# A fused attention, Fourier, MLP and gated-convolution kernel: the MLP and the value layer on three token blocks of 512 in place of four of 384

## The chip, the cores and the metric

The kernel runs on one core of one Trainium2 chip. The metric is the device time of one execution in microseconds; lower is better.

## The reference, cut to what matters

```python
# 1. causal linear attention with decay, B=2, H=8, S=768, head size 64, chunked
x = attention(q, k, v, lam)                    # (2, 768, 512)
# 2. Fourier mixing, layer norm, MLP
u = x + real(fft(fft(x, axis=1), axis=2))
mu = u.mean(-1); var = ((u - mu) ** 2).mean(-1)
un = (u - mu) / sqrt(var + 1e-6)
y = u + maximum(un @ w_ch1, 0) @ w_ch2         # w_ch1 512x2048, w_ch2 2048x512
# 3. gated convolution
gate = sigmoid(sum(conv_w[k] * shifted(y, k) for k in range(5)))
out = (gate * (y @ w_val)) @ w_out             # (2, 768, 512)
```

There are 2 x 768 = 1536 tokens and 512 features, everything in float32.

## The kernel before, in words

Features lie on the partitions (R = 4 groups of 128) and tokens along the free axis. Every product from the MLP on is made of three matmuls in a reduced form of float32: each operand is split into a high part and a low part (what the high part leaves over), and high x high, high x low and low x high add up in PSUM. ScalarE makes the high parts (a cast), GpSimd the low parts of the weights (`tensor_tensor` subtract), VectorE most of the other low parts.

The work on TensorE falls into stages, in the order in which the program lists them; each engine has its own instruction list and they meet at semaphores.

- Attention of 12 chunks of 128 tokens (6 per batch), with the Fourier transform of batch 0 in between (`hid_transform`, `seq_pair`, `radix4`, `add_pair`).
- `mean(0)`, then `centre` (VectorE subtracts the mean), `cen_hi` (ScalarE) and `cen_lo` (half on VectorE, half on GpSimd) make the MLP's input for batch 0, `cen_h` and `cen_l`.
- The MLP. The 2048 hidden features are worked off in NG = 8 weight groups of 256. A step m is one weight group on one block of TB = 384 tokens (half a batch): `mlp_hidden` has 24 matmuls into PSUM banks 0 and 1, `mlp_out` 24 matmuls into banks 4 to 7, one bank for each R. There are 32 steps, batch 0 first. The two halves of a batch take turns so that a weight group serves two steps; TensorE issues `mlp_hidden` of step m+1 before `mlp_out` of step m. ScalarE applies the Relu (L770) and VectorE makes the low part of the hidden features (L1049) from the same bank. Since the half changes every second step, banks 4 to 7 are emptied every second step: VectorE adds them onto `xT` in SBUF (`add_mlp`, L1064 and L1066).
- Normalization is moved behind the MLP: `finish_mlp` multiplies the sum by 1/std (`rstd`, L337) and adds `u` (L341). `rstd` comes from `squares`, `square_sum`, `variance`, `inverse_roots` and `newton`, spread over the steps, as is the Fourier transform of batch 1 (`hid_transform` 10 and 11, `seq_pair`, `add_pair`, `mean(1)`).
- `value` (48 matmuls for each block of 384 tokens, banks 0 to 3), `gated` (VectorE multiplies by the gate), and `project`, whose moving operand is 512 columns of `w_out` and whose stationary one is 128 tokens.

A weight group is 1 MB in two transfers of 512 KB into `raw_a` or `raw_b`, is split by ScalarE (L735) and GpSimd (L1242) into `w1h`, `w1l`, `w2h`, `w2l` (two buffers, `_a` and `_b`), and is loaded again for batch 1: 16 loads in all. SyncE issues every transfer of the weights and waits for the splits that free the buffer. The batch-1 buffers and `raw_b` overlap the attention's buffers and are free only after the last chunk.

Of the kernel before, what the change touches and what calls it, by code (L numbers as in the profile page):

```python
# [8 lines left out]
F32 = mybir.dt.float32  # L9
# [4 lines left out]
P = 128  # L14
# [3 lines left out]


Step = namedtuple("Step", "m g slot tb rnd first last new fresh")  # L20
# [36 lines left out]
def program(nc, qkv, lam, w_mlp, w_val, conv_w, w_out, seq_tab, hid_tab, out):  # L57
# [13 lines left out]
    TB = S // 2  # L71
    NB = B * 2
    STEPS = 2 * NG
    M = B * STEPS
# [4 lines left out]
    assert (P, Dh, NC, R, K) == (128, 64, 6, 4, 5)  # L79

    with ExitStack() as ctx:
# [28 lines left out]
        cen_h0 = sb("cen_h0", [P, R, S], F32R)  # L110
        cen_l0 = sb("cen_l0", [P, R, S], F32R)
# [14 lines left out]
        with ExitStack() as second:  # L126
# [6 lines left out]
            cen_h1 = sb_in(second, "cen_h1", [P, R, S], F32R)  # L133
        sb("region1_rest", [P, 6 * 2048 + R * PAD])
# [22 lines left out]
        with ExitStack() as second_l:  # L157
            cen_l1 = sb_in(second_l, "cen_l1", [P, R, S], F32R)
# [8 lines left out]
        cen_h, cen_l = [cen_h0, cen_h1], [cen_l0, cen_l1]  # L167
# [18 lines left out]
        s_raw = [sem(f"s_raw{i}") for i in range(2)]  # L186
        s_wh, s_wl = sem("s_wh"), sem("s_wl")
        s_h, s_hh, s_hl, s_ch, s_add, s_scl, s_y = (
            sem(n) for n in ("s_h", "s_hh", "s_hl", "s_ch", "s_add", "s_scl", "s_y"))
# [4 lines left out]

        HID_AT = {0: (10,), 1: (11,)}
        RADIX_AT = {0: (11,)}
# [56 lines left out]
        def group_splits(s):  # L255
            r_ = raw[s]
            half = R * FG
            return [(r_[:, 0:half].rearrange("p (r f) -> p r f", r=R), w1h[s][:, :, :], w1l[s][:, :, :]),
                    (r_[:, half:2 * half].rearrange("p (j r c) -> p j r c", j=2, r=R), w2h[s][:, :, :, :],
                     w2l[s][:, :, :, :])]  # L260

        def value_splits():
            return [(raw[0][:, kk * D:(kk + 1) * D].rearrange("p (r c) -> p r c", r=R), wvh[:, kk], wvl[:, kk])
                    for kk in range(R)]
# [5 lines left out]


        def out_pieces(o):
            if o < NB * 3 - 1:
# [3 lines left out]
        def out_splits():  # L277
            return [(raw[1][:, kk * D:(kk + 1) * D], wo_part(kk, 0), wo_part(kk, 1)) for kk in range(R)]

        GS = len(group_splits(0))  # L280
        GROUPS = B * NG
        AFTER_G = GS * GROUPS
        AFTER_V = AFTER_G + R
        AFTER_O = AFTER_V + R
# [9 lines left out]
        ROUNDS = steps[-1].rnd + 1  # L294
        added_at = {st.tb: st.rnd + 1 for st in steps}
        done_at = {st.tb: st.m + 1 for st in steps}

        def each_step(run):
            for st in steps:
                run(st, steps[st.m + 1] if st.m + 1 < M else None)  # L300

        def tok_half(t, b, hf):
            return t[b][:, :, hf * TB:(hf + 1) * TB]

        def gated_parts(tb):
            if tb == 0:
                return [t[:, :, :, :].rearrange("p a j n -> p (a j) n") for t in (hh, hl)]
            b, hf = divmod(tb - 1, 2)
            return [tok_half(t, b, hf) for t in (cen_h, cen_l)]
# [16 lines left out]

        def finish_mlp(tb, api, eng):

            tt = api.tensor_tensor
            b, hf = divmod(tb, 2)  # L330
            acc, y = tok_half(acc_of, b, hf), tok_half(u, b, hf)
# [1021 lines left out]
```

## Time and profile before

| | |
|---|---|
| median of 3 runs | 432.52 us (432.51 to 433.49) |
| the profiled execution | 432.88 us |
| its span, first to last instruction | 431.1 us |
| TensorE / VectorE / ScalarE / GpSimd busy | 99% / 59% / 37% / 33% |
| MLP steps, first to last matmul | 76.4 to 361.1 us |
| value and projection | 361.1 to 428.5 us |

The busy share of TensorE counts overlapping matmuls, each of which is shown for longer than the distance to the next, so the table tells that it is never idle for long and not how fast it is fed. The distance between the starts of two matmuls is what adds up to the time.

### The profile page before, as it was taken

The numbers are of one execution on the slowest core, as the hardware profiler recorded it, in microseconds if no ns is written. First come the engines' busy times: TensorE is split into PE (matmuls) and PEld (weight loads), VectorE is DVE, ScalarE is ACT, GpSimd is POOL, SyncE is SP. The second block draws the span as 40 slices with busy tenths as digits, with TensorE's granted clock in tenths as the row PEclk, the third lists the DMA queues.
The fourth block names the chain that finished last, engine by engine and source line by source line (L and its number), as shares of the span: only waits on it lengthen the run. The fifth ranks groups of instructions, "written<-read, shape, count | busy, mean of one in ns | idle before, by whom it ended". The sixth has DMA issues, their size and how long they took to land.

```text
span 431.1 us, 7174 instructions
## 1 busy us (share of the span) xinstructions
PE 426.3 (99%) x2914; PEld 409.1 (95%) x2914; DVE 253.1 (59%) x438; ACT 157.5 (37%) x312; POOL 143.6 (33%) x101
## 2 busy tenths in 40 slices
PE   8999999999999999999999999999999999999997
PEld 7888888999999999999999999999999999989986
DVE  5658999682359535435334239937556559899120
ACT  2355843742222411124333163542342261715222
POOL 2553321585332225224664522342242291000000
PEclk9999999999999999999999999999999999999999
DMA  7997501240220302030220211302203200001112
GB/s 232 370 320 236 178 2 51 84 152 10 97 81 18 99 0 99 0 99 1 100 94 5 97 34 65 99 3 96 97 2 97 99 0 2 1 2 73 73 50 97
DMA packets 12560, 35.73 MB, mean 83 GB/s; under 512 B 1648, under 2 KB 1904, under 8 KB 12528
## 3 DMA queue, kind: packets, MB, share of 16 engines
q1 hardware_dynamic: 12528, 35.28, 24.1%
q8 instruction: 23, 0.38, 0.4%
q14 instruction: 9, 0.07, 0.1%
HBM read 32.13 MB, written 3.15 MB: 82 GB/s over the span
## 4 chain that ended last, share of the span: by engine, by line
PE 94%; DVE 3%; DMA 2%; SPq 1%; issue 0%; ACT 0%; DVEq 0%
PE ps L556 10%; PE ps L558 10%; PE ps L579 10%; PE ps L578 10%; PE ps L577 10%; PE ps L557 10%; PE ps L650 3%; PE ps L652 3%; PE ps L651 3%; PE ps L674 3%; PE ps L672 3%; PE ps L673 3%; PE ps L427 3%; PE ps L465 2%; PE ps L454 2%; DMA chunks<-in_qkv 2%
## 5 line engine op out<-in xcount | busy, mean ns | idle before, releaser
L770 ACT ACTIVATE hh<-ps 128x384 fp32r<-128x384 f32 x64 | 31.4, 494 | 170.8 <-PE ps L558 170.8
L1049 DVE SCALAR_TENSOR_TENSOR hl<-ps,hh 128x384 fp32r<-128x384 f32 x64 | 35.2, 556 | 90.5 <-ACT hh L770 90.5
L556 PE MATMUL ps<-cen_h,w1h_a 128*128 128x384 f32 x128 | 43.8, 342 | 0.0
L556 PE MATMUL ps<-cen_h,w1h_b 128*128 128x384 f32 x128 | 43.6, 341 | 0.0
L558 PE MATMUL ps<-cen_h,w1l_b 128*128 128x384 f32 x128 | 43.2, 337 | 0.0
L579 PE MATMUL ps<-hh,w2l_b 128*128 128x384 f32 x128 | 43.1, 337 | 0.0
L578 PE MATMUL ps<-hl,w2h_b 128*128 128x384 f32 x128 | 43.1, 337 | 0.0
L577 PE MATMUL ps<-hh,w2h_b 128*128 128x384 f32 x128 | 43.1, 337 | 0.0
L558 PE MATMUL ps<-cen_h,w1l_a 128*128 128x384 f32 x128 | 43.1, 337 | 0.0
L557 PE MATMUL ps<-cen_l,w1h_a 128*128 128x384 f32 x128 | 43.1, 337 | 0.0
L557 PE MATMUL ps<-cen_l,w1h_b 128*128 128x384 f32 x128 | 43.0, 336 | 0.0
L577 PE MATMUL ps<-hh,w2h_a 128*128 128x384 f32 x128 | 42.9, 335 | 0.0
L578 PE MATMUL ps<-hl,w2h_a 128*128 128x384 f32 x128 | 42.9, 335 | 0.0
L579 PE MATMUL ps<-hh,w2l_a 128*128 128x384 f32 x128 | 42.9, 335 | 0.0
L1066 DVE TENSOR_TENSOR xT<-xT,ps 128x384 f32<-128x384 f32 x56 | 30.6, 553 | 17.8 <-PE ps L579 17.7
L1123 DVE SCALAR_TENSOR_TENSOR xT<-u_pad,cw,xT 128x768 f32<-128x768 f32 x32 | 37.9, 1243 | 0.0
L1242 POOL TENSOR_TENSOR w2l_a<-raw_a,w2h_a 128x1024 fp32r<-128x1024 f32 x8 | 19.2, 2402 | 43.1 <-ACT w2h_a L735 43.1
L1242 POOL TENSOR_TENSOR w2l_b<-raw_b,w2h_b 128x1024 fp32r<-128x1024 f32 x8 | 19.5, 2439 | 41.4 <-ACT w2h_b L735 41.4
L1242 POOL TENSOR_TENSOR w1l_b<-raw_b,w1h_b 128x1024 fp32r<-128x1024 f32 x8 | 19.9, 2489 | 38.6 <-ACT w1h_b L735 38.6
L1242 POOL TENSOR_TENSOR w1l_a<-raw_a,w1h_a 128x1024 fp32r<-128x1024 f32 x8 | 20.9, 2619 | 28.6 <-ACT w1h_a L735 28.6
L556 PEld LDWEIGHTS ps<-cen_h,w1h_a 128*128 128x128 f32 x128 | 24.1, 188 | 0.5 <-POOL cen_l L1249 0.3
L557 PEld LDWEIGHTS ps<-cen_l,w1h_b 128*128 128x128 f32 x128 | 24.3, 190 | 0.1
(169 smaller groups left out, 1002.3 us busy)
## 6 DMA issues: line engine op xcount, KB each, us to landing
raw_a<-in_mlp SPq DMA_DIRECT2D x16, 512.0 KB, 4.7
raw_b<-in_mlp SPq DMA_DIRECT2D x16, 512.0 KB, 4.4
chunks<-in_qkv SPq DMA_DIRECT2D x12, 512.0 KB, 6.4
chunks<-in_qkv SPq DMA_DIRECT2D x22, 256.0 KB, 5.7
out<-out_sb SPq DMA_DIRECT2D x11, 256.0 KB, 2.0
raw_a<-in_val SPq DMA_DIRECT2D x2, 512.0 KB, 4.4
raw_b<-in_out SPq DMA_DIRECT2D x2, 512.0 KB, 4.4
seq_c<-const_seq SPq DMA_DIRECT2D x1, 768.0 KB, 7.6
```

Of the source, the lines that this page charges most:

```text
L427: m = mm(score_bank(n, par)[:, hp * P:(hp + 1) * P], kT[c][rows, hp, :], qT[c][rows, hp, :], start=True, stop=True)
L556: mm(bank, wh_, xh, start=r == 0, stop=False)
L557: mm(bank, wh_, xl, start=False, stop=False)
L558: m = mm(bank, wl_, xh, start=False, stop=r == R - 1)
L577: mm(bank, w2h[st.slot][:, j, r], hh[:, slot, j], start=st.first and j == 0, stop=False)
L578: mm(bank, w2h[st.slot][:, j, r], hl[:, slot, j], start=False, stop=False)
L579: m = mm(bank, w2l[st.slot][:, j, r], hh[:, slot, j], start=False, stop=st.last and j == 1)
L770: nc.scalar.activation(hh[:, slot, j], ps[j][:, 0:TB], ACT.Relu).then_inc(s_hh, 1)
L1049: stt(hl[:, slot, j], ps[j][:, 0:TB], 0.0, hh[:, slot, j].bitcast(F32), ALU.max, ALU.subtract).then_inc(s_hl, 1)
L1066: tt(acc[:, r], acc[:, r], ps[4 + r][:, 0:TB], ALU.add).then_inc(s_add, 1)
L1123: stt(xT[:, b, r], u_pad[b][:, r, PAD - d:PAD - d + S], cw[:, K - 1 - d, r:r + 1], xT[:, b, r], ALU.mult, ALU.add).then_inc(s_tap, 1)
L1242: tt(lo, r_, hi.bitcast(F32), ALU.subtract).then_inc(s_wl, 1)
```

## The change

The 1536 tokens are cut into three blocks of 512, across the border between the batches: block 0 is the first 512 tokens of batch 0, block 1 the last 256 of batch 0 and the first 256 of batch 1, block 2 the last 512 of batch 1. What works by batch (mean, centring, squares, sigmoid, convolution) goes by four pieces of 512, 256, 256 and 512 tokens. A block goes through all eight weight groups alone, so there are 24 steps of 48 matmuls with 512 columns. Banks 4 to 7 add up over all eight steps of a block and are emptied once, by `finish`, which multiplies by `rstd` on the way. Each step has a weight group of its own, so 24 groups are loaded and split in place of 16, with separate semaphores and waits for the first and the second half of a group. The value layer has 3 blocks of 48 matmuls with 512 columns in place of 4 with 384. The projection has the same 144 matmuls' worth of tiles, now four tiles for each block. The work of batch 1's Fourier transform and of the normalization is spread over other steps.

```diff
-    TB = S // 2
-    NB = B * 2
-    STEPS = 2 * NG
-    M = B * STEPS
+    TB = 4 * P
+    NB = B * S // TB
+    M = NB * NG
+    LAST = M - 1
...
         def step(m):
-            b, i = divmod(m, STEPS)
-            hf = ((i + 1) // 2 + b) % 2
-            return Step(m, m // 2, m // 2 % 2, 2 * b + hf, (NG + 1) * b + (i + 1) // 2,
-                        i % 2 == 1 or i == 0, i % 2 == 0 or i == STEPS - 1, i < 2, i < 3)
+            tb, g = divmod(m, NG)
+            return Step(m, g, m % 2, tb, g == 0, g == NG - 1)
...
+        def piece(b, hf):
+            ends = (0, TB * (b + 1) - S * b, S)
+            first, end = ends[hf], ends[hf + 1]
+            tb, at = divmod(b * S + first, TB)
+            return Piece(b, slice(first, end), tb, slice(at, at + end - first))
...
@@ sync
+            def load_first(m):
+                cols, s = slice(0, R * FG), raw1_slot(m)
+                if m == 1 or m >= 3:
+                    sp.wait_ge(s_w1h, max(m - 1, 1))
+                    sp.wait_ge(s_w1l, max(m - 1, 1))
+                sp.dma_start(raw[s][:, cols], w_mlp[m % NG][:, cols]).then_inc(s_raw1[s], 16)
+            def load_second(m):
+                cols = slice(R * FG, 2 * R * FG)
+                if m >= 2:
+                    sp.wait_ge(s_w2h, m - 1)
+                    sp.wait_ge(s_w2l, m - 1)
+                sp.dma_start(raw[m % 2][:, cols], w_mlp[m % NG][:, cols]).then_inc(s_raw2[m % 2], 16)
...
+                if n == 10:
+                    load_first(1)
             sp.wait_ge(s_pv, N)
             wait_keys(sp, N - 1)
-            load_group(1, 1)
-            for g in range(2, GROUPS):
-                sp.wait_ge(s_wh, GS * (g - 1))
-                sp.wait_ge(s_wl, GS * (g - 1))
-                load_group(g % NG, g % 2)
+            for m in range(2, M):
+                load_first(m)
+                load_second(m - 1)
+            load_second(LAST)
...
@@ tensor, mlp_hidden and mlp_out
-                if st.m % 2 == 0:
-                    pe.wait_ge(s_wh, GS * st.g + 1)
-                    pe.wait_ge(s_wl, GS * st.g + 1)
+                pe.wait_ge(s_w1h, st.m + 1)
+                pe.wait_ge(s_w1l, st.m + 1)
                 for j in range(2):
-                    bank = ps[j][:, 0:TB]
+                    bank = ps[j]
...
-                    if st.m >= 1 and st.first:
-                        pe.wait_ge(s_add, R * (st.rnd - 1) + r + 1)
-                    bank = ps[4 + r][:, 0:TB]
+                    if st.first and st.tb:
+                        pe.wait_ge(s_fin, finished(st.tb - 1, r))
+                    bank = ps[4 + r]
...
@@ scalar
-            split_group(0, 1)
-            cen_hi(0, 0)
-            cen_hi(0, 1)
+            second_hi(0)
+            cen_hi(0)
+            first_hi(1)
             hidden_hi(steps[0])
             spectrum_copy(NC + 2)
             spectrum_copy(NC + 3)
-            squares(0, 0)
-            squares(0, 1)
+            first_hi(2)
+            cen_hi(1)
...
                 if after:
                     hidden_hi(after)
+                if st.m + 1 < M:
+                    second_hi(st.m + 1)
+                if st.m + 3 < M:
+                    first_hi(st.m + 3)
...
@@ vector
-            def add_mlp(st):
...
+            def finish(tb):
...
                 for r in range(R):
-                    dve.wait_ge(s_ch, R * st.m + r + 1)
...
+                    dve.wait_ge(s_ch, R * (NG * (tb + 1) - 1) + r + 1)
+                    for i in pieces_of[tb]:
+                        tt(of_batch(acc_of, i)[:, r], ps[4 + r][:, pieces[i].at], rstd[:, pieces[i].b, pieces[i].tok],
+                           ALU.mult).then_inc(s_fin, 1)
+                for i in pieces_of[tb]:
+                    for e in range(2):
+                        pair = slice(2 * e, 2 * e + 2)
+                        dve.wait_ge(s_fin, finished(tb, 2 * e + 1))
+                        tt(of_batch(u, i)[:, pair], of_batch(u, i)[:, pair], of_batch(acc_of, i)[:, pair],
+                           ALU.add).then_inc(s_y, 1)
...
@@ gpsimd
             cen_lo(0)
+            first_lo(1)
+            second_lo(0)
+            first_lo(2)
             cen_lo(1)
...
+            for m in range(M):
+                if m + 1 < M:
+                    second_lo(m + 1)
+                if m + 3 < M:
+                    first_lo(m + 3)
...
+                if m == LAST - 1:
+                    for kk in range(R):
+                        pool.wait_ge(s_wvh, kk + 1)
+                        raw_, hi, lo = value_split(kk)
+                        tt(lo, raw_, hi.bitcast(F32), ALU.subtract).then_inc(s_wvl, 1)
...
-    nc = _bacc.Bacc("TRN2", target_bir_lowering=False, num_devices=1)
+    nc = _bacc.Bacc("TRN2", target_bir_lowering=False, num_devices=1, dynamic_dma_scratch_size=1024)
```

## Rows read from the trace of the kernel before

**Rows 1.** The page: busy times, and the chain that ended last.

```profile
PE 426.3 (99%) x2914; PEld 409.1 (95%) x2914; DVE 253.1 (59%) x438; ACT 157.5 (37%) x312; POOL 143.6 (33%) x101
...
PE 94%; DVE 3%; DMA 2%; SPq 1%; issue 0%; ACT 0%; DVEq 0%
```

**Rows 2.** Busy us by stretch: TensorE, weight loads, VectorE, ScalarE, GpSimd; clock; DMA share.

```profile
76.40:361.10 284.70, 284.68 (x1663) 283.62 (x1661) 155.54 (x239) 97.79 (x155) 115.94 (x59) 1.00 0.18 60
361.10:428.50 67.40, 67.40 (x349) 61.51 (x348) 39.31 (x59) 23.58 (x38) 0.00 (x0) 1.00 0.12 44
```

**Rows 3.** Timeline of TensorE in the MLP: start, length, line, product.

```profile
217.55 0.33 PE L577 MATMUL ps<-hh,w2h_b 128*128 128x384 f32 x1
...
221.71 0.34 PE L556 MATMUL ps<-cen_h,w1h_a 128*128 128x384 f32 x1
...
264.43 0.34 PE L556 MATMUL ps<-cen_h,w1h_a 128*128 128x384 f32 x1
...
348.40 0.34 PE L556 MATMUL ps<-cen_h,w1h_b 128*128 128x384 f32 x1
```

**Rows 4.** Timeline of TensorE in value and projection, at the stages' borders.

```profile
361.10 0.34 PE L650 MATMUL ps<-cen_h,wvh 128*128 128x384 f32 x1
...
378.06 0.39 PE L672 MATMUL ps<-w1h_a,hh 128*128 128x512 f32 x1
...
386.23 0.34 PE L650 MATMUL ps<-cen_h,wvh 128*128 128x384 f32 x1
...
394.71 0.39 PE L672 MATMUL ps<-w1h_a,cen_h 128*128 128x512 f32 x1
...
403.09 0.34 PE L650 MATMUL ps<-cen_h,wvh 128*128 128x384 f32 x1
```

**Rows 5.** Timeline of all engines where the MLP begins.

```profile
72.56 1.56 PE L522 MATMUL ps<-out_sb,ones 128*128 128x384 f32 x4 [0.36 <-DVE out_sb L325]
...
73.51 1.82 DVE L1019 TENSOR_TENSOR xT<-u_pad,ps 128x768 f32<-128x768 f32 x2 [1.01 <-PE ps L522]
...
73.96 0.61 PE L485 MATMUL ps<-hid_c,zin 128*128 128x128 f32 x4
...
74.50 1.70 ACT L761 CAST cen_h<-xT 128x768 fp32r<-128x768 f32 x2 [0.71 <-DVE xT L1019]
...
75.36 0.96 DVE L1042 TENSOR_TENSOR cen_l<-xT,cen_h 128x768 fp32r<-128x768 f32 x1
...
76.27 2.00 POOL L1249 TENSOR_TENSOR cen_l<-xT,cen_h 128x384 fp32r<-128x384 f32 x2 [5.34 <-ACT cen_h L761]
...
76.42 0.49 PE L556 MATMUL ps<-cen_h,w1h_a 128*128 128x384 f32 x1
...
76.75 0.34 PE L557 MATMUL ps<-cen_l,w1h_a 128*128 128x384 f32 x1
```

**Rows 6.** Timeline of TensorE behind the mean of batch 1.

```profile
187.95 0.63 PE L556 MATMUL ps<-cen_h,w1h_a 128*128 128x384 f32 x1
188.42 0.34 PE L557 MATMUL ps<-cen_l,w1h_a 128*128 128x384 f32 x1
```

**Rows 7.** Groups by line and form: xcount, busy us, mean ns, idle before.

```profile
L1049 DVE SCALAR_TENSOR_TENSOR hl<-ps,hh 128x384 fp32r<-128x384 f32 x64 | 35.2, 556 | 90.5 <-ACT hh L770 90.5
L770 ACT ACTIVATE hh<-ps 128x384 fp32r<-128x384 f32 x64 | 31.4, 494 | 170.8 <-PE ps L558 170.8
L1066 DVE TENSOR_TENSOR xT<-xT,ps 128x384 f32<-128x384 f32 x56 | 30.6, 553 | 17.8 <-PE ps L579 17.7
...
L1242 POOL TENSOR_TENSOR w1l_a<-raw_a,w1h_a 128x1024 fp32r<-128x1024 f32 x8 | 20.9, 2619 | 28.6 <-ACT w1h_a L735 28.6
...
L735 ACT CAST w1h_a<-raw_a 128x1024 fp32r<-128x1024 f32 x8 | 8.3, 1042 | 0.0
...
L1242 POOL TENSOR_TENSOR wvl<-raw_a,wvh 128x512 fp32r<-128x512 f32 x4 | 6.6, 1670 | 5.5 <-ACT wvh L735 5.5
```

**Rows 8.** DMA issues: count, size, median us from issue to landing.

```profile
raw_a<-in_mlp SPq DMA_DIRECT2D x16, 512.0 KB, 4.7
```

More of the change, by code:

```diff
@@ L15 @@
 EPS = 1e-6
-Step = namedtuple("Step", "m g slot tb rnd first last new fresh")
+Step = namedtuple("Step", "m g slot tb first last")
+Piece = namedtuple("Piece", "b tok tb at")
 def fourier_constants(S, D):
@@ L253, in program, with raw1_slot, raw1_landed, raw2_landed @@
         out_d = out.rearrange("b (c p) n -> b c p n", p=P)
[L255 to L264, printed above, removed]
+        def raw1_slot(m):
+            return max(m - 1, 0) % 2
+        def raw1_landed(m):
+            return 16 * (m // 2 if raw1_slot(m) else (m + 1) // 2 + 1)
+        def raw2_landed(m):
+            return 16 * (m // 2 + 1)
+        def first_split(m):
+            r_ = raw[raw1_slot(m)][:, 0:R * FG].rearrange("p (r f) -> p r f", r=R)
+            return r_, w1h[m % 2][:, :, :], w1l[m % 2][:, :, :]
+        def second_split(m):
+            r_ = raw[m % 2][:, R * FG:2 * R * FG].rearrange("p (j r c) -> p j r c", j=2, r=R)
+            return r_, w2h[m % 2][:, :, :, :], w2l[m % 2][:, :, :, :]
+        def value_split(kk):
+            return raw[0][:, kk * D:(kk + 1) * D].rearrange("p (r c) -> p r c", r=R), wvh[:, kk], wvl[:, kk]
         def wo_part(kk, lo):
@@ new lines, in program, with of_batch, of_block, wide @@
+        pieces = [piece(b, hf) for b in range(B) for hf in range(2)]
+        pieces_of = [[i for i, pc in enumerate(pieces) if pc.tb == tb] for tb in range(NB)]
+        through = [max(i_s) + 1 for i_s in pieces_of]
+        def of_batch(t, i):
+            return t[pieces[i].b][:, :, pieces[i].tok]
+        def of_block(t, i):
+            return t[pieces[i].tb][:, :, pieces[i].at]
+        def wide(i):
+            cols = slice(0, pieces[i].tok.stop - pieces[i].tok.start)
+            return ps[(COS, SIN)[i % 2]][:, cols]
@@ L551, in mlp_hidden @@
                     for r in range(R):
[L552 to L553 removed]
+                        if st.first and j == 0 and r >= 2:
+                            pe.wait_ge(s_cenl[1], 2 * through[st.tb] + r - 3)
                         wh_, wl_ = (w[st.slot][:, r, j * P:(j + 1) * P] for w in (w1h, w1l))
[L555 to L558 removed]
+                        xh, xl = (x_[st.tb][:, r] for x_ in (cen_h, cen_l))
+                        mm(bank[:, :], wh_, xh, start=r == 0, stop=False)
+                        mm(bank[:, :], wh_, xl, start=False, stop=False)
+                        m = mm(bank[:, :], wl_, xh, start=False, stop=r == R - 1)
                     m.then_inc(s_h, 1)
@@ L681, in _ @@
             project(1)
-            value(3)
             project(2)
-            project(3)
         @block.scalar
@@ L873, in store @@
             def store(tb):
-                for t in range(3):
-                    o = tb * 3 + t
+                for t in range(TB // P):
+                    o = tb * TB // P + t
                     if o >= 2:
@@ L1105, in _, with taps @@
             hidden_sum(0, 3, nc.vector, dve)
-            for hf in range(2):
-                centre(0, hf)
-                cen_lo(0, hf)
+            centre(0)
+            cen_lo(0)
+            centre(1)
             hidden_lo(steps[0])
-            radix4(NC + 4)
-            def taps(b, two, d):
-                at = TAPS * (b * R + two) // 2 + 2 * (d - 1)
+            cen_lo(1)
+            radix4(N - 2)
+            radix4(N - 1)
+            def taps(n, two, d):
+                b, tok = GATES[n]
+                at = TAPS * (n * R + two) // 2 + 2 * (d - 1)
                 if two == 0 and d == 1:
@@ L1199, in _ @@
                 for d in range(1, K):
-                    taps(1, two, d)
-            for tb in (2, 3):
-                gated(tb)
-                gate_lo(tb)
+                    taps(2, two, d)
+            gated(2)
+            gate_lo(2)
         @block.gpsimd
```

515 lines of the change are left out of this document (250 added, 265 removed).

## The prediction

> **What bounds the kernel now.** I read the page first. TensorE is busy 99% of the span and has 94% of the chain that ended last [rows 1]; no other engine passes 59%. So the time is the sum of the distances between matmul starts, plus what TensorE loses where a stage begins. The second view is the busy time by stretch: the MLP takes 284.7 us, value and projection 67.4 us, at a granted clock of 1.00, the 2.4 GHz level, with TensorE never idle [rows 2]. An edit that takes work from VectorE, ScalarE or GpSimd inside these stretches is worth nothing by itself; one that changes the number of matmuls or their spacing is worth what it says there. The third view is TensorE's own timeline, for the spacing. From 264.43 to 348.40 us lie ten steps, 480 matmuls of 384 columns: 83.97 / 480 = 174.9 ns each [rows 3]. The 1536 matmuls of the 32 steps at that spacing make 268.7 us of the 284.7; the rest is the Fourier transform of batch 1 and the variances, whose number of columns doesn't change.
>
> **How the spacing depends on the width.** This decides the sum, so it is worked out before anything else. A matmul of 384 columns has no single spacing. The 24 of one `mlp_out` run from 217.55 to 221.71 us, 173.3 ns each [rows 3]; the 96 of the first two `value` blocks from 361.10 to 378.06 us, 176.7 ns each [rows 4]. The MLP's average of 174.9 ns lies 0.48 of the way between them. For 512 columns the projection has two values as well: 36 matmuls from 378.06 to 386.23 us, 226.9 ns, and 36 from 394.71 to 403.09 us, 232.8 ns [rows 4]. They differ in the tiles that are read, not in shape. Low against low, 128 more columns cost 53.6 ns, or 0.419 ns a column, which is the 2.4 GHz clock; that leaves 173.3 - 384 x 0.419 = 12.5 ns that every matmul pays whatever its width. High against high it is 56.1 ns and leaves 8.4 ns. Exactly in proportion to the columns, 174.9 ns would become 233.2 ns, and there would be no gain at all. So the MLP's new spacing lies between 226.9 and 232.8 ns. I take the point that is as far up as the MLP is today, 226.9 + 0.48 x 5.9 = 229.7 ns. The projection is another product, with the weights as the moving operand, but it is the only row with 512 columns, and the closest.
>
> A rule of the Trainium skill speaks against the change. TensorE: Matmul & The Clock Gate, "Wait — 56ns, not 53.3ns?", gives a fixed cost of about 2.5 ns for each matmul beside its columns. The trace doesn't agree with it for these products, with 12.5 ns or 8.4 ns. If 2.5 ns were all that is fixed and the rest grew with the columns, the MLP would come to some 232.4 ns a matmul and save 1 us, which is rival B below.
>
> **The change part by part.**
>
> MLP matmuls. 24 steps x 48 = 1152 of 512 columns for 1536 of 384. 1152 x 229.7 ns = 264.6 us against 268.7 us: -4.1 us. Bounds: 261.4 us at 226.9 ns (-7.3) and 268.2 us at 232.8 ns (-0.5).
>
> Value matmuls. 144 for 192. Today they are at the high spacing, 192 x 176.7 ns = 33.9 us. I keep them at the high one, 144 x 232.8 = 33.5 us: -0.4 us, down to -1.3 us at the low one. The projection keeps its 144 tiles and its width. Its first block may change from low to high or the others from high to low; I take nothing, between +0.2 us and -0.6 us.
>
> The start of the MLP. The first block needs 512 tokens ready, not 384, and this lies on the path. Today `mean` starts at 72.56, its first product (0.7 us of the 1.4 us up to 73.96) releases `centre` at 73.51, two pairs take 1.82 us, `cen_lo` 0.96 us, and the first MLP matmul starts at 76.42 [rows 5]. A third more tokens: mean +0.23 us, centre 1.82 to 2.4 us, `cen_lo` 0.96 to 1.3 us. That gives a start near 77.5 us, where the two `hid_transform` that fill the wait today end at 76.4. GpSimd's two `cen_lo` grow from 1.0 us to 1.3 us each and end near 80.0 us, 0.4 us after the matmuls want the last one; against that, 0.33 us for the first matmul and a smaller gap behind it, 0.3 us in all, stand there already. Sum +1.2 us; between +0.5 and +2.5 us.
>
> The mean of batch 1. Today the matmul behind it starts 0.47 us before its successor in place of 0.17 us [rows 6]. Now `mean(1)` stands ahead of `mlp_out(5)`, for which everything is ready: -0.3 us, or nothing.
>
> Twice as many weight groups for each step. Each step now needs a group of its own, 24 in place of 16. A step lasts 48 x 229.7 ns = 11.0 us. GpSimd has two subtractions of up to 2.6 us in it, 5.2 us; ScalarE two casts of 1.04 us and two Relus, which grow from 0.49 to some 0.65 us, 3.4 us [rows 7]; SyncE two transfers that land after 4.7 us [rows 8]. All are covered by 11.0 us of matmuls, and the transfer of a half is asked for as soon as its buffer's last split is through, a good step ahead of the cast that reads it. If the cover were gone, each microsecond of lateness would be one on TensorE. There are two narrow places. The first is group 1 for step 1: behind its `cen_lo`, GpSimd splits it from 80.0 to 82.6 us, and `mlp_hidden(0)` ends near 83.4 us: 0.8 us to spare. The second is `value(0)`, which waits for all four low parts of `w_val`: from the end of `mlp_hidden(23)` on, Relu and cast end after 1.8 us, GpSimd's last weight split after 4.4 us, four subtractions of 1.67 us [rows 7] after 11.1 us; TensorE needs 11.0 us for the two `mlp_out` before it. I cost both at nothing, at most 1 us together.
>
> VectorE. The 56 additions of 0.553 us [rows 7] and the copies beside them go, and the scaling too; 16 multiplications that read the bank and scale at once come in. It hides behind matmuls before and after. What remains to check is the block border: `finish` must free bank 4 while TensorE does the next `mlp_hidden` (5.5 us), and a multiplication of 512 columns is estimated at 0.7 us from 0.553 us for 384. It doesn't stall. At the border all of them come before `hidden_lo` of the next step, together some 5 us, which also has 5.5 us to go. Moving Fourier work forward to steps 0 to 4 loads VectorE with up to some 10 us in one step (step 1, of 11.0 us), and `hidden_lo` is needed only after the following `mlp_out`, 5.5 us later, so nothing behind it on VectorE's queue makes TensorE wait. Behind the last MLP step the convolution now covers 512 tokens and not 768 and ends sooner than it did.
>
> The rest. Loading group 1 during chunk 10 of the attention puts 512 KB ahead of chunk 11 on SyncE's queue, when little is moving. No transfer of the trace is issued by GpSimd, so the smaller scratch size costs nothing.
>
> **Sum.** -4.1 - 0.4 + 1.2 - 0.3 = -3.6 us. The profiled execution took 432.88 us, of which 431.1 us is the span and 1.8 us lie around it; so 429.3 us. The median of the runs is 0.36 us below the profiled one, and the forecast against it is 432.52 - 3.6 = 428.9 us.
>
> **Rivals.**
>
> B: the spacing grows in proportion. For it: the high row, 232.8 ns, which three of the four projection stretches have; against it: the MLP's 384-column matmuls are not at their own high value. All at 232.8 ns: -0.5 - 0.4 + 1.2 - 0.3 = 0, so 432.5 us, no change.
>
> C: the new tiles fall on the low spacing throughout. Then -7.3 - 1.3 + 1.2 - 0.3 = -7.7 us, 424.8 us. One projection stretch and several `mlp_out` show it, but the MLP never as a whole.
>
> D, slower: the wide product costs more than in proportion. The 512-column row was measured with other operands; in the MLP both streams, moving tokens and weights, could meet more often. It decides from 233.8 ns on: (1152 + 144) x 233.8 ns = 303.0 us against 268.7 + 33.9 = 302.6 us, plus 0.9 us for the start and the mean, which is 1.3 us slower. At 236 ns it would be 305.9 us, or +4.2 us: 436.7 us. Against it: no row is above 232.8 ns.
>
> E, slower too: the weights come late in every step because cast, subtraction and transfer queue behind other work on GpSimd and ScalarE. A lateness of 0.25 us in each of 24 steps is 6 us, 434.9 us. Against it: 5.2 us of work in 11.0 us.
>
> **How the numbers follow.** The forecast A has a chance of 0.58, B 0.22, C 0.08, D 0.06, E 0.06. A measurement of this kernel can tell about 0.3%, 1.3 us, from no change. Faster by more: most of A (0.54) and C (0.08), 0.62. Within: B and the rest of A, 0.26. Slower: D and E, 0.12. The range reaches from the low spacing for most of the MLP's matmuls, 425.5 us, to rival B with a late start, 433.6 us.
>
> **What would show it.** In the profile after, the spacing within `mlp_hidden` and `mlp_out` of 512 columns should be 227 to 233 ns, near 229.7; the first MLP matmul should start near 77.5 us, with a wait for `cen_lo` behind it; no gap of TensorE should stand at steps 1, 8, 16 or ahead of `value(0)`; GpSimd should be busy some 38 us more and VectorE less than today. The forecast is wrong if the spacing is above 232 ns, if TensorE waits for a weight split in each step, or if the start costs more than 2.5 us.

## The result, and the profile after

The changed kernel is slower: 446.53 us (median of 4 runs, 444.99 to 446.86) against 432.82 us for the kernel before in the same session (4 runs), a ratio of 1.031 (95% interval 1.028 to 1.034). Forecast were 428.9 us and at most 433.6 us. The profiled execution took 446.64 us with a span of 444.7 us, 13.6 us longer than the span before; the forecast was 3.6 us shorter.

From the page: busy times, slices of TensorE and of its granted clock, and the chain that ended last.

```profile
PE 427.1 (96%) x2482; PEld 352.9 (79%) x2482; DVE 260.2 (59%) x370; ACT 173.8 (39%) x318; POOL 193.5 (44%) x117
...
PE   8999999968968999999999999999999999999997
...
PEclk9999999986997999999999999999999999999999
...
PE 82%; DVE 11%; DMA 2%; SPq 1%; issue 1%; ACT 1%; POOL 1%; DVEq 0%
```

VectorE has 11% of the chain where it had 3% [rows 1], though its busy share is 59% as before. TensorE is no longer full in slices 9, 10, 12 and 13 of 40, some 89 to 111 and 122 to 145 us, and the granted clock dips in slices 9, 10 and 13. Everything else is as full as it was. So the loss sits in MLP steps 0 to 3, and the rest can be compared with the forecast by itself.

TensorE's timeline at the borders of the MLP's even part, of `value` and of `project`.

```profile
181.85 0.39 PE L574 MATMUL ps<-cen_h,w1h_b 128*128 128x512 f32 x1
...
225.91 0.28 PE L555 MATMUL ps<-square_part,ones_r 128*128 128x256 f32 x1
...
226.60 0.39 PE L574 MATMUL ps<-cen_h,w1h_b 128*128 128x512 f32 x1
...
359.17 0.39 PE L574 MATMUL ps<-cen_h,w1h_b 128*128 128x512 f32 x1
...
375.80 0.39 PE L672 MATMUL ps<-cen_h,wvh 128*128 128x512 f32 x1
...
397.60 0.39 PE L694 MATMUL ps<-w1h_a,hh 128*128 128x512 f32 x1
...
408.49 0.39 PE L672 MATMUL ps<-cen_h,wvh 128*128 128x512 f32 x1
...
419.58 0.39 PE L694 MATMUL ps<-w1h_a,cen_h 128*128 128x512 f32 x1
```

From 181.85 to 359.17 us lie 16 steps, 768 matmuls. Without the 0.69 us of the variances at 225.91 that is 176.63 / 768 = 230.0 ns each. The 96 `value` matmuls from 375.80 to 397.60 us run at 227.1 ns, the 48 from 408.49 to 419.58 us at 231.0 ns. The MLP's spacing is as forecast, and the value layer's a little below its forecast of 232.8 ns.

TensorE's timeline at the three waits (start, length, line, product, in brackets the idle time and what ended it).

```profile
94.14 0.39 PE L596 MATMUL ps<-hh,w2l_a 128*128 128x512 f32 x1
96.55 0.68 PE L507 MATMUL ps<-hid_c,zin 128*128 128x128 f32 x4 [2.02 <-DVE zin L997]
...
97.50 0.82 PE L509 MATMUL ps<-hid_c,zin 128*128 128x256 f32 x2
101.92 1.20 PE L507 MATMUL ps<-hid_c,zin 128*128 128x128 f32 x4 [3.59 <-DVE zin L997]
...
128.68 0.39 PE L596 MATMUL ps<-hh,w2l_a 128*128 128x512 f32 x1
134.66 0.55 PE L532 MATMUL ps<-seq_c,yy 128*128 128x128 f32 x1 [5.59 <-DVE yy L1066]
```

`hid_transform(10)` waits for `zin`, `hid_transform(11)` for the next `zin`, and `seq_pair(1,0)` for `add_eps` (L1066), which stands behind `third_pair(1)` and `hidden_lo(3)` on VectorE's queue. By distances between starts, less the usual spacing, they cost 2.2, 4.0 and 5.75 us, 11.9 us in all.

Busy time by stretch: stretch, its length, busy us of TensorE, weight loads, VectorE, ScalarE and GpSimd, granted clock, DMA share, GB/s.

```profile
88.90:104.25 15.35, 9.74 (x41) 7.54 (x40) 15.17 (x13) 6.16 (x10) 13.30 (x9) 0.79 0.30 103
104.25:111.68 7.43, 7.43 (x27) 5.92 (x25) 0.69 (x1) 1.52 (x6) 0.00 (x0) 0.75 0.00 0
123.40:139.30 15.90, 10.31 (x51) 9.02 (x49) 12.40 (x17) 5.06 (x7) 5.48 (x2) 0.79 0.31 101
```

The stretch from 88.90 to 104.25 us holds the first two waits; VectorE is busy in 15.17 of its 15.35 us. The second row is `mlp_hidden(2)`, which waits for nobody: 7.43 us for 24 matmuls that take 5.5 us elsewhere, at a granted clock of 0.75; in its first 3 us the granted clock is 0.50, the 1.2 GHz level, and the matmuls start 427 ns apart. In the same way `hid_transform(11)` takes 2.33 us in place of 1.3, and `seq_pair(1,0)` 4.60 in place of 2.6. So 1.0 + 1.9 + 2.0 = 4.9 us are lost to the clock. It was still 1.00 when the first wait ended, fell at some 97.7 us, behind the few products between the first two waits, and fell again at some 131.9 us, within the third.

VectorE's timeline over the first two waits.

```profile
91.54 2.50 DVE L996 TENSOR_TENSOR zin<-esum 128x128 f32<-128x128 f32 x1
93.96 2.44 DVE L997 TENSOR_TENSOR zin<-esum 128x128 f32<-128x128 f32 x1
96.50 2.38 DVE L991 TENSOR_TENSOR esum<-xT 128x256 f32<-128x256 f32 x1
...
101.49 0.28 DVE L997 TENSOR_TENSOR zin<-esum 128x128 f32<-128x128 f32 x1
101.69 1.27 DVE L1088 SCALAR_TENSOR_TENSOR hl<-ps,hh 128x512 fp32r<-128x512 f32 x2
```

GpSimd's timeline over the same stretch.

```profile
91.29 2.60 POOL L1295 TENSOR_TENSOR w2l_b<-raw_b,w2h_b 128x1024 fp32r<-128x1024 f32 x1
93.84 2.41 POOL L1290 TENSOR_TENSOR w1l_b<-raw_a,w1h_b 128x1024 fp32r<-128x1024 f32 x1
96.21 2.40 POOL L1308 TENSOR_TENSOR yy<-yy 128x1024 f32<-128x1024 f32 x1
...
101.50 0.86 POOL L1310 TENSOR_TENSOR yy<-yy 128x256 f32<-128x256 f32 x1
```

The same addition of 128 columns, L997, takes 2.44 us at 93.96 and 0.28 us at 101.49. Lay the two lists side by side. Each long VectorE instruction begins while one of GpSimd runs and ends 0.15 to 0.3 us after it: GpSimd's end at 93.89, 96.25 and 98.61 us, VectorE's at 94.04, 96.40 and 98.88. The length of the VectorE instruction says nothing about its own work. The two L1088, of which one input is a PSUM bank, begin beside GpSimd's addition of 101.50 us and take 1.27 us together; at 132.31 us, where GpSimd is idle, two of them take 1.28 us. This is what the Trainium skill says (SBUF — State Buffer, "Who interferes with whom"): a VectorE instruction with two SBUF inputs and a GpSimd one that reads SBUF exclude each other for the whole of the one that came first, and one with at most one SBUF input, outside the modes that use two ports, isn't touched. The trace agrees, with 0.28 us that become 2.44 us.

The third wait has the same form. From 113.12 to 132.4 us VectorE works off the 14 additions of `chunk_pair`, `two_even`, `two_odd` and `third_pair`; at 0.68 us apiece they would take 9.5 us. Five of them take 2.33 to 2.93 us, each beside a GpSimd instruction. One such pair, from VectorE's and from GpSimd's timeline:

```profile
120.72 2.93 DVE L1007 TENSOR_TENSOR sd<-yy 128x514 f32<-128x514 f32 x1
```

```profile
120.20 2.90 POOL L1290 TENSOR_TENSOR w1l_a<-raw_b,w1h_a 128x1024 fp32r<-128x1024 f32 x1
```

### The profile page after: what moved, and what is told of

Read it like the earlier page. It is cut to its first block, busy times and chain, and to the rows that moved or that the text cites. A ratio compares the mean times of both kernels' runs of the same rounds, so it can differ in the third digit from the quotient of the medians.

```text
span 444.7 us, 6312 instructions
## 1 busy us (share of the span) xinstructions
PE 427.1 (96%) x2482; PEld 352.9 (79%) x2482; DVE 260.2 (59%) x370; ACT 173.8 (39%) x318; POOL 193.5 (44%) x117
## 4 chain that ended last, share of the span: by engine, by line
PE 82%; DVE 11%; DMA 2%; SPq 1%; issue 1%; ACT 1%; POOL 1%; DVEq 0%
PE ps L574 9%; PE ps L575 9%; PE ps L576 9%; PE ps L594 9%; PE ps L595 9%; PE ps L596 9%; PE ps L694 2%; PE ps L695 2%; PE ps L696 2%; PE ps L672 2%; PE ps L673 2%; PE ps L674 2%; PE ps L449 2%; DMA chunks<-in_qkv 2%; PE ps L487 2%; PE ps L476 2%
## 5 line engine op out<-in xcount | busy, mean ns | idle before, releaser
L1088 DVE SCALAR_TENSOR_TENSOR hl<-ps,hh 128x512 fp32r<-128x512 f32 x48 | 32.7, 688 | 110.4 <-ACT hh L801 110.4
L1169 DVE SCALAR_TENSOR_TENSOR xT<-u_pad,cw,xT 128x768 f32<-128x768 f32 (+2 forms) x48 | 56.0, 1235 | 0.0
L1295 POOL TENSOR_TENSOR w2l_b<-raw_b,w2h_b 128x1024 fp32r<-128x1024 f32 x12 | 30.3, 2521 | 54.9 <-ACT w2h_b L768 54.9
L574 PE MATMUL ps<-cen_h,w1h_a 128*128 128x512 f32 x96 | 39.1, 407 | 0.8 <-issue 0.6
L594 PE MATMUL ps<-hh,w2h_b 128*128 128x512 f32 x96 | 38.4, 400 | 0.0
L575 PE MATMUL ps<-cen_l,w1h_a 128*128 128x512 f32 x96 | 38.2, 398 | 0.0
L576 PE MATMUL ps<-cen_h,w1l_a 128*128 128x512 f32 x96 | 38.1, 397 | 0.0
L596 PE MATMUL ps<-hh,w2l_b 128*128 128x512 f32 x96 | 37.8, 394 | 0.0
L595 PE MATMUL ps<-hl,w2h_b 128*128 128x512 f32 x96 | 37.8, 394 | 0.0
L575 PE MATMUL ps<-cen_l,w1h_b 128*128 128x512 f32 x96 | 37.7, 392 | 0.0
L574 PE MATMUL ps<-cen_h,w1h_b 128*128 128x512 f32 x96 | 37.6, 392 | 0.0
L576 PE MATMUL ps<-cen_h,w1l_b 128*128 128x512 f32 x96 | 37.6, 391 | 0.0
L1290 POOL TENSOR_TENSOR w1l_a<-raw_b,w1h_a 128x1024 fp32r<-128x1024 f32 x11 | 30.6, 2782 | 2.3 <-ACT w1h_a L761 2.3
```

Source lines behind the costliest of these rows:

```text
L574: mm(bank[:, :], wh_, xh, start=r == 0, stop=False)
L575: mm(bank[:, :], wh_, xl, start=False, stop=False)
L576: m = mm(bank[:, :], wl_, xh, start=False, stop=r == R - 1)
L594: mm(bank[:, :], w2h[st.slot][:, j, r], hh[:, slot, j], start=st.first and j == 0, stop=False)
L595: mm(bank[:, :], w2h[st.slot][:, j, r], hl[:, slot, j], start=False, stop=False)
L596: m = mm(bank[:, :], w2l[st.slot][:, j, r], hh[:, slot, j], start=False, stop=st.last and j == 1)
```

## The experiments

Ten kernels were run, each beside the kernel before, whose median was 433.01 us with the first four, 432.72 us with the next four and 432.88 us with the last two. The expectations name their theories themselves; T1 is the one above: GpSimd's long instructions hold up VectorE's queue, TensorE waits for it, and the waits cost clock behind them.

**e1_short_pool: take the long GpSimd instructions away.** The work of GpSimd in the early steps is cut to a few columns, and so leaves that part of the low parts and sums out. The cut below leaves out the same edit of `squares_lo(0)` and two copies on ScalarE, which fill tiles that would stay unwritten.

```diff
 @@ first_lo
+                if 3 <= m <= 5:
+                    raw_, hi, lo = (t[:, :, 0:8] for t in (raw_, hi, lo))
...
 @@ second_lo
+                if 1 <= m <= 3:
+                    raw_, hi, lo = (t[:, :, :, 0:8] for t in (raw_, hi, lo))
...
 @@ square_sum
+                if i < 2:
+                    t = t[:, :, 0:8]
```

> This kernel leaves work out: GpSimd's low parts of the weights of steps 1 to 3 (second half) and 3 to 5 (first half), its sums of squares of batch 0 and their low part are made for a few columns only. Semaphores, order and VectorE's own instructions are those of the changed kernel. Theory T1 (contention): VectorE's instructions that read two operands from SBUF stand still while a GpSimd subtraction runs (0.28 us becomes 2.4 us in the changed kernel's trace), and that makes TensorE wait three times, 2.0, 3.6 and 5.6 us, with some 5 us more for the granted clock that falls behind the gaps. Then these VectorE instructions are back at 0.28 to 0.7 us, the three gaps are under 1 us together, the granted clock is 1.00 and the time is 429 to 431 us. Rival T2 (order and amount): the Fourier work moved into steps 0 and 1 is too much for VectorE's queue by itself. Then at least two of the gaps stay, over 5 us together, and the time is 440 us or more.

429.54 us (429.19 to 429.86), ratio 0.992 (0.991 to 0.994), granted clock 0.999. VectorE's timeline, and then TensorE's, where the first wait was:

```profile
91.24 0.28 DVE L1000 TENSOR_TENSOR zin<-esum 128x128 f32<-128x128 f32 x1
91.44 0.42 DVE L1001 TENSOR_TENSOR zin<-esum 128x128 f32<-128x128 f32 x1
```

```profile
93.85 0.39 PE L596 MATMUL ps<-hh,w2l_a 128*128 128x512 f32 x1
94.08 0.60 PE L507 MATMUL ps<-hid_c,zin 128*128 128x128 f32 x4
```

All three waits are gone with the length of GpSimd's instructions, and with them the loss of clock. VectorE's program is the same as in the changed kernel.

**e2_turns: keep all the work, and let the two engines take turns.** GpSimd waits with its next weight splits until `radix4(11)` and, later, `third_pair(1)` are through.

```diff
             for m in range(M):
+                if m == 0:
+                    pool.wait_ge(s_r4, R4 * N)
                 if m + 1 < M:
                     second_lo(m + 1)
+                if m == 1:
+                    pool.wait_ge(s_r6, R6 * B)
                 if m + 3 < M:
                     first_lo(m + 3)
```

> All work is done. GpSimd waits with second_lo(1) until VectorE's last radix4 is through, and with first_lo(4) until the last operation of third_pair is through; nothing else is changed. T1 (contention): the first two gaps (2.0 and 3.6 us) go, the third shrinks from 5.6 to at most 2 us because two GpSimd instructions still fall into VectorE's chain of step 1; the time is 431 to 436 us. Rival T2 (order and amount): VectorE's queue is as long as before and GpSimd is later besides, so the time is 445 us or more.

429.87 us (429.64 to 430.11), ratio 0.993 (0.991 to 0.994), below the 431 to 436 us that were expected. GpSimd's timeline, then VectorE's:

```profile
93.39 2.38 POOL L1295 TENSOR_TENSOR w2l_b<-raw_b,w2h_b 128x1024 fp32r<-128x1024 f32 x1 [2.04 <-DVE zin L997]
...
117.21 2.43 POOL L1290 TENSOR_TENSOR w1l_a<-raw_b,w1h_a 128x1024 fp32r<-128x1024 f32 x1 [6.20 <-DVE yy L1029]
```

```profile
93.03 0.28 DVE L997 TENSOR_TENSOR zin<-esum 128x128 f32<-128x128 f32 x1
```

GpSimd gives up 2.04 us in the first turn and 6.20 us in the second, which it has to spare, and TensorE gets back 16.7 us: the 11.9 us of waits and the 4.9 us of clock to 0.1 us. T1 had allowed for a rest of the third wait; there is none, although two of VectorE's additions in that chain still take 2.33 and 2.88 us. This is the changed kernel as it should have been, at the 428.9 us of the forecast within 1 us.

**e6_first_turn: the first turn alone.** The edit is e2's without its second half, the wait on `s_r6`.

> The changed kernel with the first turn alone: GpSimd's second_lo(1) waits for the last radix4; nothing holds first_lo(4) back in step 1. T1: the two waits ahead of hid_transform are gone with the fall of the clock behind them (2.1 + 4.0 + 1.0 + 1.9 = 9.0 us), and the wait ahead of seq_pair(1,0) is there as long as VectorE's chain of step 1 is lengthened by three GpSimd instructions: 1 to 4 us with up to 2 us for the clock. 432 to 437 us. If the second gap only came from the first two (VectorE late from step 0 on), the time is that of both turns, 430 us.

438.11 us (437.78 to 439.71), ratio 1.013 (1.011 to 1.015), so a little above the range. TensorE's only wait on VectorE of over 0.4 us behind the start of the MLP (waited in total, times, longest), and VectorE's timeline before it:

```profile
PE ps L532 <- DVE yy L1066: 6.0, 1, 6.0
```

```profile
107.18 2.33 DVE L1014 SCALAR_TENSOR_TENSOR yy<-sd 128x514 f32<-128x514 f32 x1
109.44 2.88 DVE L1018 TENSOR_TENSOR yy<-sd 128x514 f32<-128x514 f32 x1
112.24 2.94 DVE L1019 SCALAR_TENSOR_TENSOR yy<-sd 128x514 f32<-128x514 f32 x1
...
119.13 2.86 DVE L1025 TENSOR_TENSOR yy<-sd 128x514 f32<-128x514 f32 x1
```

The first two waits don't bring about the third; it has five encounters of its own (L1024 with 2.78 us is left out above), which add 1.7 to 2.3 us each, and isn't shortened by an earlier start. Each turn mends its own place: 446.53 to 438.11 us by the first, to 429.87 us by the second.

**e3_fill and e7_fill_half: keep TensorE busy in the waits.** To price the clock by itself, products nobody needs fill the waits: 16, 30 and 46 of them, then 9, 16 and 23.

```diff
+            def fill(bank, products):
+                for _ in range(products):
+                    mm(ps[bank][:, 3 * P:4 * P], ones[:, :], ones[:, :], start=True, stop=True)
...
                 if st.m == 0:
+                    pe.wait_ge(s_cen, 4)
+                    fill(COS, 16)
                     hid_transform(N - 2)
+                    fill(SIN, 30)
                     hid_transform(N - 1)
                 if st.m == 2:
+                    for _ in range(46):
+                        mm(ps[7][:, 3 * P:4 * P], ones[:, :], ones[:, :], start=False, stop=False, skip_group_check=True)
                     seq_pair(1, 0)
```

> The changed kernel with TensorE given small products of ones to do while it waits: 16 and 30 of 128 columns ahead of hid_transform(10) and hid_transform(11), 46 ahead of seq_pair(1,0) (these add a small constant to 128 columns of one accumulating bank, so the output is changed by that). Theory: the granted clock fell because TensorE stood idle, and it costs 1.9 us in mlp_hidden(2), 2.0 us in seq_pair(1,0) and 1.0 us in hid_transform. Then the granted clock stays at 1.00, the waits for VectorE stay as long as they are, and the time is 441 to 442.5 us. Rival: the clock falls for another reason, or its cost is hidden behind the waits that follow; then the time stays within 1.5 us of 446.5 us.

450.47 us (449.97 to 450.52), ratio 1.040 (1.039 to 1.042), slower than the changed kernel. The expectation had the products end inside the waits. TensorE's timeline:

```profile
94.62 3.73 PE L635 MATMUL ps<-ones 128*128 128x128 f32 x32
...
98.19 0.61 PE L507 MATMUL ps<-hid_c,zin 128*128 128x128 f32 x4
```

The 16 products are 32 records and take 3.57 us, 0.22 us each, for a wait of 2.2 us. All three fillings, 20.6 us, outlast the waits, and the time is e2's plus 20.6 us to 0.1 us. The granted clock stayed at 1.00, but as a price of the clock this run says nothing; e7, with about half as many products, was made for that.

> As the run with the waits filled, but with 9, 16 and 23 products, since one took 0.22 us on TensorE there and the 92 filled 20.6 us, more than the waits. Now they take 2.0, 3.6 and 5.2 us and end inside the waits. Theory: the granted clock stays at 1.00 and that gives back 4.5 to 5 us, 441.5 to 442.5 us. Rival: nothing is given back, since the clock's cost is hidden; 446.5 us.

442.38 us (441.22 to 442.51), ratio 1.022 (1.020 to 1.023), granted clock 1.00. TensorE's timeline at the first wait:

```profile
94.69 2.17 PE L635 MATMUL ps<-ones 128*128 128x128 f32 x18
96.86 0.68 PE L507 MATMUL ps<-hid_c,zin 128*128 128x128 f32 x4
```

The distances at the three places are those of the changed kernel (2.2, 4.0 and 5.7 us over the spacing), now filled for the most part, and the clock doesn't fall. Against the changed kernel it is 4.2 us less, where the sum of the three stretches had given 4.9 us; against e2 it is 12.5 us more, where the waits had given 11.9 us. So the two parts of the loss are shown apart, with some 0.6 us between them that the fillers themselves may cost.

**e4_later and e8_later_lo_first: is it the earlier place of the Fourier work?** A rival theory lays the loss on batch 1's Fourier work having been moved into steps that are too full. In e4 it comes one or two steps later on all engines, with no turns.

```diff
 tensor
-                if st.m == 0:
+                if st.m == 1:
                     hid_transform(N - 2)
                     hid_transform(N - 1)
-                if st.m == 2:
-                    seq_pair(1, 0)
...
+                if st.m in (4, 5):
+                    seq_pair(1, 2 * (st.m - 4) + 1)
...
 vector
-                if st.m == 0:
-                    chunk_pair(1, 0)
                 if st.m == 1:
+                    chunk_pair(1, 0)
+                if st.m == 2:
+                    add_eps(0)
+                    add_eps(1)
                     chunk_pair(1, 1)
```

> All work is done. The same instructions, with batch 1's Fourier work one or two steps later: hid_transform(10), (11) behind mlp_out(1), VectorE's chain of 16 operations split over steps 1, 2 and 3, seq_pair(1, 0..3) in steps 4 and 5, mean(1) in step 6. GpSimd's splits run as before. T1 (contention): VectorE's instructions are still lengthened where they meet GpSimd (some at over 2 us), but TensorE doesn't wait for them; no gap over 1 us in steps 0 to 7, granted clock 1.00, 429 to 432 us, which is below the kernel before by 0.3% or more. If the spacing of the matmuls had cost the time and not the waits, it would stay at 440 us or more.

439.92 us (439.53 to 440.29), ratio 1.016 (1.014 to 1.018), a miss by 8 us. It is also near the 440 us that the expectation gave to the spacing of the matmuls, but the trace shows a wait. VectorE's timeline, then TensorE's:

```profile
91.86 2.50 DVE L992 TENSOR_TENSOR zin<-esum 128x128 f32<-128x128 f32 x1
...
101.99 1.27 DVE L1084 SCALAR_TENSOR_TENSOR hl<-ps,hh 128x512 fp32r<-128x512 f32 x2
```

```profile
94.47 0.39 PE L596 MATMUL ps<-hh,w2l_a 128*128 128x512 f32 x1
102.81 0.77 PE L574 MATMUL ps<-cen_h,w1h_a 128*128 128x512 f32 x1 [7.96 <-DVE hl L1084]
```

TensorE no longer needs `zin` here, yet it waits 8 us, more than the first two waits together, now for `hidden_lo(1)` (L1084), which frees the PSUM banks and stands behind the two `radix4` on VectorE's queue. Moving the consumer was not enough. e8 is e4 with `radix4(10)` and `radix4(11)` behind `hidden_lo(1)` (shown against the changed kernel):

```diff
             cen_lo(1)
-            radix4(N - 2)
-            radix4(N - 1)
...
                 if st.m == 0:
+                    radix4(N - 2)
+                    radix4(N - 1)
```

> The later order of batch 1's Fourier work, and radix4(10) and (11) on VectorE behind hidden_lo(1) in place of ahead of it. GpSimd works as in the changed kernel, without turns. In the later order one wait of 8.3 us was left, ahead of mlp_hidden(2), which needs hidden_lo(1), which stood behind the lengthened radix4 on VectorE. T1: VectorE's instructions are still lengthened beside GpSimd (up to 2.4 us), but now no matmul waits for them; no gap over 1 us in steps 0 to 7, granted clock 1.00, 429 to 431 us, as with turns. If the lengthening itself were needed for the loss whatever the order, a gap of 3 us or more would show elsewhere and the time be 434 us or more.

429.93 us (429.26 to 430.50), ratio 0.993 (0.992 to 0.995). VectorE's timeline:

```profile
91.98 2.63 DVE L990 TENSOR_TENSOR zin<-xT 128x256 f32<-128x256 f32 x1
94.53 2.48 DVE L992 TENSOR_TENSOR zin<-esum 128x128 f32<-128x128 f32 x1
```

The long encounters are still there, here and in the later chain (up to 2.89 us), and cost TensorE nothing, since it waits for nothing behind them: no wait on VectorE of over 0.4 us, at a granted clock of 1.00. The 10.0 us between e4 and e8 are e4's wait of 8.1 us and the clock behind it. So this rival holds half: a later place is a cure, too, but only with an order of VectorE's queue that allows for 2.5 us where 0.3 us are nominal.

**e5_aligned, e10_alike and e9_before_aligned: the spacing.** In the changed kernel the spacing depends on the buffer: in block 1 `mlp_hidden` takes 229.8 ns with `w1h_a` and 227.5 with `w1h_b`, `mlp_out` 227.2 with `w2h_a` and 233.0 with `w2h_b`. In block 2, with other tokens' tiles, `mlp_hidden` with `w1h_b` is at 232.1. e5 is e2 with every tile that the matmuls read starting at a multiple of 512 bytes in its partition.

```diff
-        cw = sb("cw", [P, K, R])
...
-        u_pad0 = sb("u_pad0", [P, R, PAD + S])
...
+            cen_h2 = sb_in(second, "cen_h2", [P, R, TB], F32R)
             u_pad1 = sb_in(second, "u_pad1", [P, R, PAD + S])
-            cen_h2 = sb_in(second, "cen_h2", [P, R, TB], F32R)
...
-        sb("region2_rest", [P, B * NC * YW])
+        sb("region2_rest", [P, B * NC * YW + 104])
...
+        u_pad0 = sb("u_pad0", [P, R, PAD + S])
+        cw = sb("cw", [P, K, R])
```

> All work is done. The kernel with turns, and only places in SBUF changed: conv_w's tile (80 bytes a partition) and u_pad0 (12352 bytes) are put behind everything else, u_pad1 behind cen_h2, and 416 bytes are left free behind yy, so that every operand of the MLP, value and projection matmuls begins at a multiple of 512 bytes. Theory T4 (placement): the spacing of the 512-column matmuls is 227 ns where the stationary and the moving tile start alike and 230 to 233 ns where they don't (mlp_hidden with w1h_a 229.8, mlp_out with w2h_b 233.0, both with the other buffer 227). Then all stand at 226.7 to 227.5 ns, which is 2.9 ns less on 1152 matmuls of the MLP and some 3 to 4 ns less on the value layer's last block and two thirds of the projection, 4 us together: 425.5 to 426.5 us. Rival: the spacing follows from something else (which engine runs beside it, the values), so it stays and the time is within 0.7 us of 429.9 us.

425.60 us (425.18 to 426.24), ratio 0.984 (0.982 to 0.985), the fastest of all; e10's time isn't distinct from it. TensorE's timeline:

```profile
251.70 0.39 PE L574 MATMUL ps<-cen_h,w1h_b 128*128 128x512 f32 x1
...
311.54 0.39 PE L594 MATMUL ps<-hh,w2h_b 128*128 128x512 f32 x1
```

11 halves of a step, 264 matmuls in 59.84 us: 226.7 ns each, and so in the value layer and in the projection's first block. e10 puts `cw`, 80 bytes, back ahead of all of them, so that none starts at a multiple of 512 and all are shifted alike.

> The aligned kernel with conv_w's 80 bytes put back ahead of the other tiles: all operands of these matmuls are shifted alike, so that stationary and moving tile start alike but at no multiple of 512 bytes. If only being alike matters, the spacing stays 226.7 ns and the time 425.6 us within 0.6 us. If a multiple of a power of two matters for itself, the spacing is 230 to 233 ns in all of them and the time is 430 to 433 us.

425.81 us (425.47 to 426.05), ratio 0.984 (0.982 to 0.985), spacing 226.7 ns. So for 512 columns a shift of all tiles by 80 bytes changes nothing; that they stand alike is what counts. The changed kernel fits this, if its tiles are laid one behind the other in the program's order and sizes. In blocks 1 and 2 the pairs that then start alike (`w1h_b` with `cen_h1`, `w2h_a` with `hh`) are those at 227 to 228 ns, and the pairs that don't are those at 229.6 to 233.3 ns. e9 gives the kernel before the same placement (and the smaller scratch size of the changed one, for room).

> The kernel before, with its tiles put in SBUF as in the aligned run (every operand of the MLP, value and projection matmuls at a multiple of 512 bytes); nothing else. If placement is what lies between 173.3 and 177 ns for 384 columns, all stand at 173.3 ns: 1.6 ns less on 1536 matmuls, 3.4 ns on 192 and 6 ns on 108 of the projection, 3.8 us together, 428.7 to 429.3 us, and the change of widths with turns is then worth 3 to 3.5 us on aligned tiles. Rival: placement matters only for 512 columns or only with the changed order; then the time is within 1 us of 432.7 us.

430.29 us (429.55 to 430.82), ratio 0.994 (0.992 to 0.995), 1 us above the range. TensorE's timeline:

```profile
250.68 0.33 PE L577 MATMUL ps<-hh,w2h_b 128*128 128x384 f32 x1
...
300.60 0.33 PE L577 MATMUL ps<-hh,w2h_a 128*128 128x384 f32 x1
```

12 halves of a step, 288 matmuls in 49.92 us: 173.3 ns each. With both widths free of the placement, 128 columns more cost 53.3 ns, 0.417 ns each, and 173.3 - 384 x 0.417 = 13.3 ns are fixed. The projection, at 227.8 ns, stays 1.1 ns above its spacing in e5. For 384 columns no shifted placement was run, and standing alike is not the whole account there: by the same laying out, the tiles of `mlp_out` in the kernel before stand alike with `w2h_a` and it takes 174.2 ns (from 209.18 to 213.36 us), while with `w2h_b` they don't and it takes 173.3 ns [rows 3]. With their tiles placed so, the wide version with turns stands 4.5 us below the narrow one of the same session (e10's 425.81 against 430.29 us).

## Why the prediction was wrong

The step that failed is the VectorE term: "Moving Fourier work forward to steps 0 to 4 loads VectorE with up to some 10 us in one step (step 1, of 11.0 us), and `hidden_lo` is needed only after the following `mlp_out`, 5.5 us later, so nothing behind it on VectorE's queue makes TensorE wait." It was costed at nothing and measured 11.9 us of waits and 4.9 us of clock (16.8 us; e2 gives back 16.7). It failed in three ways.

- The 10 us are nominal lengths. Beside GpSimd, which now has two long subtractions in every step, each encounter turns 0.3 or 0.7 us into 2.3 to 2.9 us (e1, e2).
- It asked what waits for `hidden_lo` and not what waits for the moved work itself: `hid_transform(10)` and `(11)` stand right behind `mlp_out(0)`, `seq_pair(1,0)` right behind `mlp_out(2)`. Those were the waits. e4 shows that `hidden_lo(1)` was late as well: with the moved work's readers out of the way, TensorE waited 8.1 us for it.
- It left out what a wait costs behind it. Rival E had priced a stall at its own length; here 11.9 us cost another 4.2 us (e7) to 4.9 us (the stretches).

The trace before had shown the effect. Groups of VectorE by line and form, of the kernel before: the same addition on the same shapes, with two means.

```profile
L954 DVE TENSOR_TENSOR zin<-esum 128x128 f32<-128x128 f32 x12 | 5.1, 422 | 0.0
L955 DVE TENSOR_TENSOR zin<-esum 128x128 f32<-128x128 f32 x12 | 3.4, 284 | 0.0
```

At 90.44 us one L952 took 2.62 us, beside a GpSimd subtraction from 90.18 to 92.77 us. It did no harm: the last `zin` was ready at 95.1 us, and `hid_transform(11)`, which reads it, stood behind one step more and began at 99.0 us. GpSimd also had 32 weight splits in the MLP and not 48. Which of the two spared the kernel before was not tried.

The other terms, as the trace after has them:

- **MLP matmuls.** 1152 x 230.0 ns = 265.0 us, -3.7 us (the spacing measured on two thirds of them); forecast -4.1 us with 229.7 ns. The way to it, 0.48 of the way between two rows, was an interpolation between what turned out to be effects of placement (e5, e10), and the closeness is luck in part. Rival B's 232.8 ns is about the spacing of one buffer of four in block 1 and of two in block 2, rival C's 226.9 ns that of all when they are placed alike; D is excluded.
- **The fixed cost of a matmul.** Forecast 12.5 ns from the low rows, measured 13.3 ns (e5, e9). The 2.5 ns that the prediction cites from the Trainium skill (TensorE: Matmul & The Clock Gate, "Wait — 56ns, not 53.3ns?") don't hold for these products.
- **Value matmuls.** 96 x 227.1 + 48 x 231.0 ns = 32.9 us, -1.0 us; forecast -0.4, inside its bounds.
- **The start.** First MLP matmul at 77.46 us, 1.0 us later than before, forecast 77.5. The first matmul and the wait for `cen_lo` behind it cost another 0.4 us, as much as they did before. Together +1.1 us for +1.2.
- **The mean.** `mean(1)` is followed by a matmul 0.63 us before its successor, 0.40 us over the spacing. Before it was 0.30 us [rows 6], so +0.1 us for -0.3 us.
- **The weights.** No wait at step 1, at steps 8 and 16 or ahead of `value(0)`: 0, as forecast, in the face of GpSimd's 193.5 us for 143.6. GpSimd was in time everywhere; what it did to VectorE was the matter. Two signs of the prediction show it: GpSimd grew by 50 us and not by 38, its weight subtractions from 2402 to 2619 ns up to 2521 to 2782 ns on average, and VectorE, which was to be busy for less, has 260.2 us for 253.1, and 242.4 us with GpSimd cut short (e1).

These five time terms make -3.5 us for the forecast's -3.6, and with 16.8 us they make +13.3 of the 13.6 us by which the span grew. The span of e2, without the waits, is 3.3 us below the one before. So the rest of the sum held, the spacing in it in part by luck. The range missed because no rival had VectorE late, and E, the nearest, had a chance of 0.06 from "5.2 us of work in 11.0 us", a sum of busy times once more.

## What to carry to other kernels

Before work is moved on one of VectorE and GpSimd, lay their two timelines side by side over the stretch where it will stand: an instruction of one that reads two SBUF tiles can take as long as the one that the other is in, so a queue of n short ones costs up to n long ones, and two groups of one shape with different means in the trace are the sign of it. Cost a moved step by asking who waits for its result and for each instruction behind it, add to stalls of TensorE of some us what the clock costs behind them, and where a stall of this kind shows, try a turn (a semaphore on the engine that has time) before anything is rescheduled. And before the width of a matmul is changed for its spacing, place the tiles of both operands at multiples of 512 bytes: that was worth 2.6 us here on the kernel before and 4.3 us on the changed one.

## What the runs showed of the hardware

- The distance between reduced-float32 matmuls depends on how the tiles they read are placed relative to one another in the partition: 226.7 ns for 512 columns when alike (e5, e10), up to 233.3 ns when not; 173.3 ns for 384 columns with all at multiples of 512 bytes (e9), up to 176.7 ns otherwise [rows 4]. Which pair of tiles has to be alike, and why, was not tried.
- A 128 x 128 product of float32 tiles takes 0.22 us in two records, about as long as a reduced-float32 matmul of 512 columns (e3).
- TensorE's waits of 4.0 and 5.75 us were each followed by products at the 1.2 GHz level, behind that of 4.0 us with matmuls of 512 columns 427 ns apart; that of 2.2 us ahead of them was not. With small products in all three waits the granted clock stayed at 1.00 (e3, e7).
- A VectorE addition of two SBUF tiles that began beside a GpSimd subtraction ended 0.15 to 0.3 us after it, 2.44 us for 0.28 us, and GpSimd's subtractions beside such additions grew from some 2.4 to 2.9 us.
